# Attention, routing and feed-forward on one core: where ScalarE rounds the next keys, and in which slot GpSimd makes its constants

## What is computed

```python
# q, k, v: (2, 8, 768, 64) float32; n_sink 4, window 128
scores = (q @ k.T) / sqrt(64)
keep = (key position < 4) or (0 <= query - key < 128)
a = softmax(where(keep, scores, -1e9))
x = a @ v                                   # as rows: (1536, 512)

# experts: w_gate (512, 8), w1 (8, 512, 1024), w2 (8, 1024, 512), 192 rows each
# (token, expert) pairs in falling order of x @ w_gate; a token takes the
# first expert that still has room
y[mask_e] = relu(x[mask_e] @ w1[e]) @ w2[e]

# feed-forward: w_in (512, 2048), w_out (2048, 512), alpha (2048)
h = y @ w_in
out = (max(h, 0) + alpha * min(h, 0)) @ w_out
```

## Time and profile before

| | before |
|---|---|
| time, median of 3 runs | 640.17 us (639.58 to 641.13) |
| span of the profiled execution | 638.6 us |
| median less this span | 1.57 us |
| TensorE matmul busy (PE) | 619.2 us, 97% |
| TensorE weight load busy (PEld) | 556.5 us, 87% |
| VectorE busy (DVE) | 418.5 us, 66% |
| ScalarE busy (ACT) | 306.8 us, 48% |
| GpSimd busy (POOL) | 197.0 us, 31% |

### The profile page before, as it was taken

How to read it: one execution, slowest core, us unless ns; L and a number is a source line. 1 busy time by engine, 2 the same in 40 slices (tenths; PEclk the granted TensorE clock), 3 DMA queues, 4 the chain that set the end, 5 groups by cost and what they waited for, 6 DMA issues and landing times.

```text
span 638.6 us, 12935 instructions
## 1 busy us (share of the span) xinstructions
PE 619.2 (97%) x4949; PEld 556.5 (87%) x4954; DVE 418.5 (66%) x1156; ACT 306.8 (48%) x716; POOL 197.0 (31%) x211
## 2 busy tenths in 40 slices
PE   8899999889999999999999999999999999999996
PEld 4788898759899888899999888999989889999995
DVE  8788787978566979854669798438587420035552
ACT  5878784511132665532236554322465642346663
POOL 5988880010111442111113331111234410113331
PEclk9999999989999999999999999999999999999999
DMA  7477764525350143027102510370016620000001
GB/s 259 150 264 265 260 203 139 210 92 200 113 227 1 67 141 133 2 84 255 52 2 73 201 66 3 116 272 1 2 67 222 240 81 19 1 1 1 1 1 50
DMA packets 31221, 72.37 MB, mean 113 GB/s; under 512 B 2876, under 2 KB 2936, under 8 KB 31160
## 3 DMA queue, kind: packets, MB, share of 16 engines
q1 hardware_dynamic: 27232, 60.69, 27.0%
q0 software_dynamic: 1984, 6.29, 3.0%
q10 hardware_dynamic: 1944, 4.56, 2.0%
HBM read 65.22 MB, written 6.32 MB: 112 GB/s over the span
## 4 chain that ended last, share of the span: by engine, by line
PE 76%; DVE 3%; DMA 1%; issue 0%; POOLq 0%; ACT 0%; POOL 0%; DVEq 0%
PE bank L1602 21%; PE bank L1617 21%; PE bank L1514 14%; PE bank L1505 13%; PE bank L1392 3%; DVE beats L971 1%; DMA rank_row<-key_row 1%; PE bank L1461 1%; PE bank L1483 1%; DVE beats L942 1%; PE bank L1445 0%; PE bank L1233 0%; DVE ties L984 0%; PE bank L1394 0%; PE bank L1438 0%
## 5 line engine op out<-in xcount | busy, mean ns | idle before, releaser
L603 POOL TENSOR_TENSOR wi_lo<-w_in,wi_hi 128x512 fp32r<-128x512 f32 x64 | 89.5, 1401 | 274.2 <-ACT wi_hi L744 274.2
L942 DVE TENSOR_SCALAR beats<-rank_row,key 128x512 bf16<-128x512 f32 (+11 forms) x144 | 91.3, 655 | 12.4 <-PE bank L1394 12.4
L1617 PE MATMUL bank<-wo_lo,g_hi 128*128 128x512 f32 x192 | 76.0, 396 | 0.0
L1617 PE MATMUL bank<-wo_hi,g_lo 128*128 128x512 f32 x192 | 75.7, 394 | 0.0
L1617 PE MATMUL bank<-wo_hi,g_hi 128*128 128x512 f32 x192 | 75.5, 393 | 0.0
L1215 DVE SCALAR_TENSOR_TENSOR g<-bank,g_neg 128x384 f32<-128x384 f32 x64 | 35.5, 554 | 52.9 <-ACT g_neg L796 52.9
L794 ACT ACTIVATE g_neg<-bank 128x384 f32<-128x384 f32 x64 | 31.4, 491 | 79.9 <-PE bank L1602 79.1
L668 ACT ACTIVATE prob<-neg_s,neg_max 128x260 f32<-128x260 f32 x96 | 48.9, 510 | 19.1 <-DVE neg_max L853 17.7
L1602 PE MATMUL bank<-y_hi,wi_hi 128*128 128x384 f32 x256 | 57.9, 347 | 0.0
L770 ACT ACTIVATE h_t<-bank 128x192 f32<-128x192 f32 x64 | 21.2, 331 | 74.3 <-PE bank L1505 74.3
L1602 PE MATMUL bank<-y_lo,wi_hi 128*128 128x384 f32 x256 | 55.2, 336 | 0.0
(11 more groups left out here) (180 smaller groups left out, 1364.6 us busy)
## 6 DMA issues: line engine op xcount, KB each, us to landing
w_a<-moe_w SPq DMA_DIRECT2D x8, 1024.0 KB, 5.0
w_a<-moe_w SPq DMA_DIRECT2D x4, 2048.0 KB, 11.4
w_b<-moe_w SPq DMA_DIRECT2D x8, 1024.0 KB, 5.1
w_b<-moe_w SPq DMA_DIRECT2D x4, 2048.0 KB, 10.5
k_raw<-k_t SPq DMA_DIRECT2D x11, 512.0 KB, 4.8
q_raw<-q_t SPq DMA_DIRECT2D x11, 512.0 KB, 3.9
w_in<-moe_w_in SPq DMA_DIRECT2D x8, 512.0 KB, 5.2
w_out<-moe_w_out SPq DMA_DIRECT2D x8, 512.0 KB, 5.2
```

Of the source, the lines that this page charges most:

```text
L603: nc.gpsimd.tensor_tensor(out=wi_lo[:, f % 2, :, :], in0=w_in[:, :, f * P:(f + 1) * P], in1=wi_hi[:, f % 2, :, :].bitcast(F32), op=ALU.sub ...
L942: return nc.vector.tensor_scalar(out=beats[:, c % 3, lo:hi], in0=rank_row[:, lo:hi], scalar1=key[:, c:c + 1], scalar2=None, op0=op)
L1617: last = nc.tensor.matmul(DOWN_BANK[t][:, :], a[:, f % 3, t * P:(t + 1) * P], w[:, f % 2, :], start=(f == 0 and n == 0), stop=(f == FC - 1 ...
```

## The change

Two edits in the attention stage, nothing else. In ScalarE's stream, the rounding of the next block's keys goes from behind the first exponential of a slot to ahead of it, and so also ahead of the waits of that exponential. In GpSimd's stream, the 18 instructions of `routing_consts` go from slot 6 to slot 11, the last one with scores. There GpSimd has no operands to make for a next slot. The wait for `qk_split` that stood ahead of them in slot 6 goes too.

```diff
@@ GpSimd's attention_slot
-                if s in (2, 4, 6):
+                if s in (2, 4):
                     pool.wait_ge(qk_split, nxt)
                 if s == 2:
                     build_mask(mask_even, 10, P, 0, True)
                 if s == 4:
                     build_mask(mask_odd, 14, 0, P, True)
-                if s == 6:
+                if s == STEPS - 1:
                     routing_consts()
@@ ScalarE's attention_slot
                 for h in range(H):
+                    if h == 0 and 1 < front + 1 < STEPS:
+                        round_next_k(front + 1)
                     if front < STEPS:
                         b = front % 2
                         act.wait_ge(maxed, H * front + h + 1)
...
                         nc.scalar.activation(prob[b][:, h, :], neg_s[:, h % 4, :], ACT.Exp,
                                              bias=neg_max[b][:, h:h + 1], scale=-1.0,
                                              accum_out=p_sum[b][:, h, 0:1]).then_inc(exped, 1)
-                    if h == 0 and 1 < front + 1 < STEPS:
-                        round_next_k(front + 1)
```

## The result

The changed kernel takes 638.58 us in the median (637.30 to 639.96, 22 runs); the kernel before, run beside it on the same chip, takes 640.14 us (639.21 to 642.27, 22 runs). The ratio is 0.9971, with a 95% interval of 0.9964 to 0.9978. So the change is faster by 0.29% of the time, 1.56 us by the medians. The forecast was 638.3 us, the range 637.2 to 639.9.

The account below looks back on a forecast made before the run. It took ordinary slots as bound by TensorE's own work at 7.65 us, with an equally long GpSimd-ScalarE loop. 1.35 + 0.33 + 0.18 = 1.86 us, so 640.17 - 1.86 = 638.3 us, range 637.2 to 639.9.

Parts of the forecast that it names:

- The constants: Slot 7, set by GpSimd end to end: without the 18 constants it falls from 9.00 to 7.65, 1.35 us; slot 11 free.
- The overlap: Slot 7: rounding alone would win about 1.4 us, constants alone 1.35, together 1.86 and not 2.8.
- The floor: Ordinary attention slots: bound by TensorE's own work at 7.65 us, so a shorter loop gives nothing there.
- the loop through GpSimd and ScalarE: Ordinary slots: q rounding, key rounding behind the first exponential, subtraction, next first scores; one turn 7.64 us, as long as TensorE's work.
- The cross-check: Slot 11, no keys to round: last products start 6.61 us behind first scores, as in slot 9 (6.62), so TensorE binds.
- slots 4 and 6: Attention slots held up by GpSimd: each falls from 7.74 to 7.65, 0.18 us for both.
- slot 5: Slot behind the building of mask_odd on GpSimd: falls from 7.98 to 7.65, 0.33 us.
- Behind attention: After attention everything hangs on the complete x, nothing is tied to program start; the whole 1.86 us arrives at the end.
- Rival 1: Clock fall shifts onto dense matmul work: 1.65 us lost, net about +1.1, 639.4 us; at best 637.7; bad side's chance 0.12.
- Rival 2: Attention slots: the rounding wins nothing, only the constants count, 638.8 us; chance 0.11.
- Rival 3: No change, 640.2 us: the gain is absorbed behind attention; chance 0.05.
- Rival 4: Slower: ScalarE waits for keys ahead of exponentials; from 8.4 us landing, each further us lost in some 8 slots; chance 0.04.

Follow-up runs that it names:

- e2: The kernel before with only the constants moved to slot 11, the rounding left behind the first exponential: 639.88 us, ratio 0.9998.
- e0: The changed kernel with both edits, unchanged, timed again beside other runs on one chip: 638.27 us, ratio 0.9974 to the kernel before.
- e1: The changed kernel with the constants put back in slot 6, so only the rounding is moved: 638.45 us, ratio 0.9980.
- e3: The changed kernel with both masks built before slot 0 instead of in slots 2 and 4: 637.21 us, ratio 0.9962.
- e6: The changed kernel with an extra GpSimd subtraction of about 1 us in each of slots 7 to 10: 638.61 us, ratio 0.9974.
- e5: The kernel before with each head's low-piece score product left out, relieving only TensorE: 639.81 us, ratio 0.9981.
- e4: The changed kernel with each head's low-piece score product left out, relieving only TensorE: 635.56 us, ratio 0.9917.
- e11: The changed kernel with extra GpSimd subtractions in slots 7 and 8, so routing starts about as late as in the kernel before: 641.28 us, ratio 1.0009.
- e7: The kernel before with an extra GpSimd subtraction of about 1 us in each of slots 7 to 10: 643.87 us, ratio 1.0057.
- e9: The changed kernel with key loads, for slot 4's keys and later, queued behind the x store, v and big-weight loads: 640.34 us, ratio 1.0009.

## Why the prediction was right, and where it was not

**The path and the total.** Right: the time 638.58 (forecast 638.3), attention as the place, GpSimd between ScalarE and TensorE as the mechanism, and the places named in advance. From the start of slot 4 on, slot 8's first scores come 30.46 us later and slot 11's 53.31; by the forecast (71.0 and 94.0 from 40.43) it should have been 30.6 and 53.6. The rounding is ahead with a gap of 0.15 us behind it, `k_lo` doesn't wait, and the constants lie between 94.98 and 97.63. The last pack is at 102.16 and the routing at 111.65, which less the late start of 0.80 is 101.4 and 110.9 (forecast 101.6 and 111.1).

**The constants, 1.35 us.** e2 shows this number in the slot where it was placed: 9.00 to 7.65. At the new place they cost nothing: from the first scores of the last slot to the routing it is 17.11 to 17.12 us in before, after, e0, e1, e2 and e3 alike.

**The overlap.** The prediction gave the rounding alone 1.4 us, with slot 7 near 8.1, from a slack of 1.2 us for GpSimd. The slack was right (1.20 to 1.22 us ahead of each pack from slot 7 to slot 11, and e6). The step that was off is that only one slot's worth of it would be spent on the constants. The pack of the middle waits for nothing when GpSimd is behind, so the constants use up two: 7.91 in e1, and 1.80 us instead of 1.4. The sum of both stays nearly the same; its division doesn't. In this kernel the second edit adds 0.30 us to the first.

**The floor, the step that failed.** "An ordinary slot is bound by TensorE's own work at 7.65 us", with the loop through GpSimd and ScalarE equally long. TensorE's own work is 7.61 to 7.62, and the loop was 7.65. The forecast had named slots below 7.6 us as proof against it, and 7.61 is just not that, but the equality it rested on is refuted by e2 (7.65 with the loop in place) against after (7.61) and by e5 (7.44, a loop with TensorE relieved) against e4 (7.03). The cross-check was slot 11, from first scores to last products 6.61 us against 6.62 in slot 9; a difference of 0.01 to 0.03 was beyond what two starts rounded to 0.01 and a modelled end can tell, and the stretch between the last products and the next first scores, where the loop closes, wasn't in it. The terms that rest on the floor were therefore all a little small: slots 4 and 6 gave 0.13 + 0.13 = 0.26 us (predicted 0.18), slot 5 gave 0.36 (0.33), slot 7 gave 1.38 (1.35), slots 8 to 10 gave 0.10 (0). Together 2.10 and not 1.86, outside the bounds of 1.68 and 1.90.

**Behind attention.** "Everything hangs on the complete x, so the gain should arrive at the end" is right in kind: where the clock is alike, 2.0 to 2.3 of 2.1 us arrive. Rival 1, the clock that falls elsewhere, was held to be one fall that is in place or not. It is rather that the share of executions with more falls rises: 0.5 us of 2.1 are lost in the medians. Two of its readings fall short. The earlier trace rows don't show TensorE lightly used while the clock is low: it is busy 6.76 of 8 us there. And it priced the fall in the routing at 0.6 us, where a second one (after) shows no cost; what the first costs no trace tells. What costs time is a further fall in the dense expert work; the rival's 1.65 us for one at its worst place is near the 1.2 to 1.5 us by which e11, e3 and e0_both are longer from the routing to the end than before. The falls in the routing come at other places from one execution to the next (114 to 126 us at 0.50 to 0.95 in e0_both, at 0.71 to 1.00 in after, at 1.00 in before). The Trainium skill (TensorE: Matmul & The Clock Gate, What's actually happening) says that the gate counts freely and doesn't start with the kernel, and the traces agree with it. That the number of falls differs between these kernels it doesn't say, and e11 contradicts both explanations that were tried. **What makes the falls more frequent stays open.** Nor do the groups prove that the clock is the cause of the time and not a companion of it; they only fit in size. The windows from 142 to 152 us are the stronger evidence, for that one place. The two errors, 0.24 us more in the slots and 0.5 less behind, are of opposite sign, and that the total came so near (1.56 us won, 1.86 forecast) is in part luck.

**The other rivals.** Rival 2 (the rounding wins nothing) is refuted by e1 and by e6 against e7. Rival 3 (no change) by the result. Rival 4 had its place right, and its threshold held in kind: with keys that land late ScalarE waits 7.3 us, and 0.9 is lost. Its price, each us beyond the slack lost in each of 8 slots, was not tested by e9, whose waits end at 1.4 us. `k_lo` takes 2.37 to 2.39 us at its new place, so the rule of the Trainium skill (SBUF — State Buffer, Who interferes with whom) that the prediction weighed made no difference in the slots.

## What to carry to other kernels

Where an engine's small step stands behind a wait it doesn't need, moving it ahead frees the engine that waits for it, and what this is worth is read from the slots that are longer than the rest: here 2.00 us from the four longer ones and 0.10 from the other three. Two edits that feed the same slack must be costed together and each by itself (1.80 and 1.33 us, together 2.10), and slack that lies in one turn of a pipeline can be carried into the next as long as the consumer runs a turn behind. When two loops look equally long to 0.01 us, one row can't tell which binds; take work from one engine in both orders of the code and compare what each gives back (0.59 us here and 0.21 there).

## What the runs showed of the hardware

The mean granted clock of one and the same kernel differs from execution to execution (0.988 to 0.997 for the kernel before), and the median differs by 1.3 us between the upper and the lower group (1.0 with both edits, 0.1 in e1, 2.2 in e2). It matters where the clock is low: in slot 1 of the after trace and as a second stretch in the routing it showed no cost, in slots 1 and 2 of e1 1.3 us, in the first expert work 1.2 to 1.5 us. A trace's win of 1.3 us (e2) can be absent from the median of 12 runs, most likely for that reason, so both must be read.

Some of GpSimd's work takes longer early in the kernel; that VectorE's work beside it is the cause was not tested: the three selects for `mask_even` take 1.88 us at the start of e3, beside VectorE's subtractions of keys and q, and 1.16 us in slot 2 of the changed kernel; GpSimd's rounding of q for slot 2 took 1.39 us in the earlier trace rows and takes 1.04 at 16.33 us in e3. But the full-size `k_lo` takes 2.36 to 2.40 us in every slot looked at, with VectorE at work in all of them.
